# Re-ordering the first batch of a fused attention, token-mixing and gated-MLP kernel, and moving one wait and some weight splits

## The reference, cut to what matters

```
state = alpha[t] * state + k[t] v[t]^T ;  y[t] = q[t] state          # attention, per head
theta = x @ w_theta ; zr = x*cos(theta) ; zi = x*sin(theta)
u  = x + w_tok_r @ zr + w_tok_i @ zi                                 # over the 768 tokens
x2 = u + relu(u @ w_ch)
h  = relu(x2 @ w_in) ; u, v = halves of h
v_n = (v - mean(v)) / sqrt(var(v) + 1e-6)
v_s = w_spatial @ v_n + b_spatial
out = (u * v_s) @ w_out
```

## Time and profile before

| | |
|---|---|
| median of 3 runs | 617.14 us |
| the profiled execution's own time | 616.59 us |
| its span, first to last instruction | 614.9 us |
| busy: TensorE / VectorE / ScalarE / GpSimd | 586.9 / 364.6 / 223.4 / 260.4 us |
| mean granted TensorE clock | 0.994 |
| TensorE idle in all | 28.0 us |
| of that before 110 us | some 22 us, 8.9 of them the start |
| of that, waits of `angles` (395) for `xT_low`, by the view of waits | 7.6 us in 5, the longest 3.0 |

### The profile page before, as it was taken

How to read it: one execution, slowest core, us unless ns; L and a number is a source line. 1 busy time by engine, 2 the same in 40 slices (tenths; PEclk the granted TensorE clock), 3 DMA queues, 4 the chain that set the end, 5 groups by cost and what they waited for, 6 DMA issues and landing times.

```text
span 614.9 us, 11189 instructions
## 1 busy us (share of the span) xinstructions
PE 586.9 (95%) x4608; PEld 556.3 (90%) x4608; DVE 364.6 (59%) x564; ACT 223.4 (36%) x411; POOL 260.4 (42%) x208
## 2 busy tenths in 40 slices
PE   3898898999999999999999999899999999999998
PEld 3687788999999999999999989898999899989997
DVE  5799688687667876877643347537233723372132
ACT  2555454443353433433443216414131323142110
POOL 5656397554353434643513036636113611362130
PEclk9999999999999999999999999799999999999999
DMA  8652111133131311421123190200220020002002
GB/s 315 219 202 102 65 65 66 66 111 122 48 121 66 104 65 66 150 80 57 51 103 116 46 341 1 77 1 2 77 78 2 1 78 1 1 0 78 0 2 78
DMA packets 20259, 49.54 MB, mean 81 GB/s; under 512 B 1648, under 2 KB 15216, under 8 KB 19696
## 3 DMA queue, kind: packets, MB, share of 16 engines
q1 hardware_dynamic: 20208, 48.81, 22.8%
HBM read 39.37 MB, written 9.44 MB: 79 GB/s over the span
## 4 chain that ended last, share of the span: by engine, by line
PE 79%; DVE 8%; ACT 4%; POOL 3%; issue 2%; DMA 2%; SPq 0%; DVEq 0%; ACTq 0%; POOLq 0%
PE psY L413 20%; PE psY L532 6%; PE psC L445 6%; PE psC L395 5%; PE psS L532 4%; PE psF L532 4%; PE psY L506 4%; PE psS L346 3%; PE psF L374 3%; PE psC L532 2%; PE psY L516 2%; PE psS L506 2%; PE psF L496 2%; DVE akq L780 2%; DVE after L771 2%
## 5 line engine op out<-in xcount | busy, mean ns | idle before, releaser
L986 POOL TENSOR_TENSOR z_lo<-cos_sin,z_hi 128x768 fp32r<-128x768 f32 x23 | 43.0, 1869 | 107.6 <-ACT z_hi L627 107.5
L1056 POOL TENSOR_TENSOR gated_lo<-u_gated,gated_hi 128x384 fp32r<-128x384 f32 x32 | 32.4, 1012 | 126.7 <-ACT gated_hi L731 126.6
L780 DVE TENSOR_TENSOR_SCAN akq<-akq,rtotal 128x516 f32<-128x516 f32 x24 | 57.1, 2381 | 0.9
L413 PE MATMUL psY<-tok_r_hi,z_hi 128*128 128x384 f32 x141 | 51.1, 362 | 2.1 <-POOL tok_i_lo L980 1.5
L969 POOL TENSOR_TENSOR akq<-akq,after 128x512 f32<-128x512 f32 x24 | 44.4, 1848 | 9.0 <-DVE after L771 7.4
L413 PE MATMUL psY<-tok_i_lo,z_hi 128*128 128x384 f32 x141 | 47.3, 335 | 0.0
L413 PE MATMUL psY<-tok_i_hi,z_lo 128*128 128x384 f32 x141 | 47.3, 335 | 0.0
L413 PE MATMUL psY<-tok_r_hi,z_lo 128*128 128x384 f32 x141 | 47.2, 335 | 0.0
L413 PE MATMUL psY<-tok_i_hi,z_hi 128*128 128x384 f32 x141 | 47.2, 335 | 0.0
L413 PE MATMUL psY<-tok_r_lo,z_hi 128*128 128x384 f32 x141 | 47.1, 334 | 0.0
L731 ACT ACTIVATE gated_hi<-u_gated 128x384 fp32r<-128x384 f32 x32 | 16.8, 525 | 82.5 <-DVE u_gated L920 82.5
(11 more groups left out here) (222 smaller groups left out, 1753.3 us busy)
## 6 DMA issues: line engine op xcount, KB each, us to landing
akq<-akq SPq DMA_DIRECT2D x23, 770.0 KB, 4.4
v<-v_in SPq DMA_DIRECT2D x24, 192.0 KB, 4.8
x_dram<-u_f SPq DMA_DIRECT2D x8, 576.0 KB, 3.7
x_raw<-x_dram SPq DMA_DIRECT2D x4, 1152.0 KB, 5.2
out<-ot SPq DMA_DIRECT2D x24, 192.0 KB, 1.9
raw_tok_r<-w_tok_rT SPq DMA_DIRECT2D x6, 384.0 KB, 7.7
raw_tok_i<-w_tok_iT SPq DMA_DIRECT2D x6, 384.0 KB, 8.9
raw_sp<-w_spT SPq DMA_DIRECT2D x1, 2304.0 KB, 9.2
```

Of the source, the lines that this page charges most:

```text
L413: mm = pe.matmul(psY[:, j, 0:HALF], Z[s][l][:, q, tile(j)], W[m][:, s, half(h)], start=(s == 0 and q == 0 and n == 0), stop=(s == CHUNKS - ...
L780: dve.tensor_tensor_scan(ALPHA[s], ALPHA[s], rtotal[:, 1:], rtotal[:, 0:1], ALU.mult, ALU.add).then_inc(decayed, 1)
L986: pool.tensor_tensor(Z[c][1][:], trigs[g % 2][:], f(Z[c][0][:]), ALU.subtract).then_inc(z_lo, 1)
L1056: pool.tensor_tensor(GA[1][:, j, half(h)], ug[h][:, j], f(GA[0][:, j, half(h)]), ALU.subtract).then_inc(g_lo, 1)
```

## The change

- First batch, VectorE: `update_state` goes ahead of `reduce_angle`, and `xT_low` ahead of `multiply_z`.
- First batch, ScalarE: `xT_high` goes ahead of `sines`, `keep_xT` ahead of `z_high`.
- First batch from chunk 1 on, GpSimd: queries are scaled before keys, so that both scalings stand behind both scans. `scores` also waits for the keys now.
- First batch, TensorE: one third of the token unit stands ahead of `transpose_x`, two thirds behind it.
- The token weights' parts 6 to 11 are split one chunk earlier (chunks 5, 6, 7 in place of 6, 7, 8), and w_ch is split ahead of the parts of its chunk.
- First MLP batch: the wait for the bias moves from ahead of all moments to the first `gate`, the moments of tiles 0 and 1 and the first `norm` go ahead of the last three `make_x2`, and all six rows of the spatial weights get their low part on VectorE (before, the last two on GpSimd).

```diff
-SPLITS = ((0, 1), (2,), (3,), (4,), (5,), (), (6, 7), (8, 9), (10, 11)) + ((),) * (BATCH * CHUNKS)
+SPLITS = ((0, 1), (2,), (3,), (4,), (5,), (6, 7), (8, 9), (10, 11)) + ((),) * (BATCH * CHUNKS)
...
                 pe.wait_ge(q_scaled, g + 1)
+                pe.wait_ge(k_scaled, g + 1)
...
                 attend(c)
-                token_mix(FIRST_UNITS[c])
+                token_mix(FIRST_UNITS[c], (0,))
                 transpose_x(c)
+                token_mix(FIRST_UNITS[c], (1, 2))
...
                         pe.wait_ge(vn_lo, b * CHUNKS + s + 1)
-                        if s < SP_VECTOR:
-                            pe.wait_ge(sp_lo, s + 1)
-                        else:
-                            pe.wait_ge(sp_lo_end, s + 1 - SP_VECTOR)
+                        pe.wait_ge(sp_lo, s + 1)
...
                 for i in SPLITS[c]:
                     tok_high(i)
+                xT_high(c)
                 if c:
                     sines(c - 1)
-                xT_high(c)
+                keep_xT(c)
                 if c:
                     z_high(c - 1)
-                keep_xT(c)
...
-                    for i in SPLITS[g]:
-                        tok_high(i)
                     if g == CHUNKS:
                         act.wait_ge(ch_in, 16)
                         act.activation(WC[0][:], raw_ch[:], ACT.Copy).then_inc(ch_hi, 1)
+                    for i in SPLITS[g]:
+                        tok_high(i)
...
                 if c:
                     decay_keys(c + 1)
                     decay_queries(c + 1)
-                    reduce_angle(c - 1)
                 update_state(c)
                 if c:
+                    reduce_angle(c - 1)
+                xT_low(c)
+                if c:
                     multiply_z(c - 1)
-                xT_low(c)
...
                 dve.wait_ge(gi_relu, n + 1)
+                if n == 0:
+                    dve.wait_ge(bias_in, 16)
...
             make_u(HALVES * b + 1)
+            find_moments(0, 0)
+            find_moments(0, 1)
+            norm(0, 0)
             for m in range(CT):
                 make_x2((HALVES * b + 1) * CT + m, last_banks[m])
 
-            dve.wait_ge(bias_in, 16)
             for b in range(BATCH):
-                find_moments(b, 0)
-                for i in range(1, CHUNKS):
+                if b:
+                    find_moments(b, 0)
+                for i in range(1 if b else 2, CHUNKS):
                     find_moments(b, i)
                     norm(b, i - 1)
                 norm(b, 5)
                 if b == 0:
-                    for c in range(SP_VECTOR):
+                    for c in range(CHUNKS):
...
                 if c:
+                    scale_queries(c + 1)
                     scale_keys(c + 1)
-                    scale_queries(c + 1)
                 for i in SPLITS[c]:
                     tok_low(i)
...
-                    for i in SPLITS[g]:
-                        tok_low(i)
                     if g == CHUNKS:
                         pool.wait_ge(ch_hi, 1)
                         pool.tensor_tensor(WC[1][:], raw_ch[:], f(WC[0][:]), ALU.subtract).then_inc(ch_lo, 1)
+                    for i in SPLITS[g]:
+                        tok_low(i)
...
                 if b == 0:
-                    for c in range(SP_VECTOR, CHUNKS):
-                        pool.wait_ge(sp_hi, c + 1)
-                        pool.tensor_tensor(WS[1][:, c, :], raw_sp[:, c, :], f(WS[0][:, c, :]),
-                                           ALU.subtract).then_inc(sp_lo_end, 1)
```

More of the change, by code:

```diff
@@ L41 @@
 VSLOTS = 3
-SP_VECTOR = 4
 SEG = P + 1
@@ L203, in build @@
         in_in, sp_in, out_in, bias_in = sems("in_in sp_in out_in bias_in")
-        in_hi, in_lo, sp_hi, sp_lo, sp_lo_end, out_hi, out_lo = sems("in_hi in_lo sp_hi sp_lo sp_lo_end out_hi out_lo")
+        in_hi, in_lo, sp_hi, sp_lo, out_hi, out_lo = sems("in_hi in_lo sp_hi sp_lo out_hi out_lo")
         x2_in, x2_hi, x2_lo = sems("x2_in x2_hi x2_lo")
```

## The result

The changed kernel takes **620.69 us** (median of 20 runs, 617.78 to 621.99) against 616.63 (20 runs, 615.31 to 619.04): ratio 1.0058, 95% interval 1.0045 to 1.007, so slower by 0.6%. The profiled execution spans 619.6 us, 4.7 more than before. The 20 runs fall in two groups: ten have a mean granted clock of 0.992 or more and a median of 618.9 us, and ten have 0.989 or less and a median of 621.6, the profiled one (621.42, 0.986) among them. The forecast was 619.0.

The account below looks back on a forecast made before the run. VectorE was taken to bound the first batch, with TensorE busy 95% of the span. 616.59 + 8.3 (first part) - 6.4 (MLP) gave 618.5, put at 619.0 us because the profiled run lies 0.55 below the median; range 612.5 to 623.5.

Parts of the forecast that it names:

- The rule that the second comer waits for the whole instruction: VectorE and GpSimd: whichever comes second waits for the other's whole instruction, if VectorE's operands are all in SBUF.
- The cycle: First batch, chunks 2, 3 and 4: the period between masks grows from 10.33 to 12.3 us.
- Chunk 1's narrow case: First batch: chunk 1's clamp, at 25.9, comes just behind the subtraction started at 25.80; next mask 1.4 us later.
- Second scan: VectorE, first batch: with no scaling beside it, the second scan takes 1.23 us against 2.10, saving 0.87.
- Thirds cost nothing: TensorE, first batch: a third of a unit ahead of the transposes costs nothing; idle before chunk 5's angles shrinks to 1.
- Parts 6 and 7: GpSimd, chunk 5: token parts ahead of chunk 4's z subtraction make unit (0,4) start at 81.5, +7.9 us.
- Chunks 6 to 8: Some waits vanish (+7.0 us); u's late split makes the channel product wait 3.5 us; unit (1,2)'s 1.27 wait goes.
- The MLP: MLP's start: earlier copies remove the spatial-weight waits and the clock's fall, -6.4 us.
- 8.3 us at that point: Unit (1,2), after chunks 6 to 8: 7.0 + 2.9 - 1.3, rounded down, makes TensorE 8.3 us later.
- the 2.95 us ahead of 70.28 did not lower the clock: TensorE, before chunk 5's angles: an earlier 2.95 us idle gap without a clock fall, cited against the clock rival.
- The rival of the clock: First batch: clock falls at TensorE's gaps, costing 3 to 4 us each; 622 once, 625 twice; chance 0.25.
- Sign: Whole kernel: no change within 0.5% (614.1 to 620.2 us) at 0.40, slower 0.40, faster 0.20.

Follow-up runs that it names:

- e4: The changed kernel with GpSimd waiting, ahead of its token subtraction in chunks 1 to 5, until that chunk's clamp is done: 617.16 us, ratio 1.0009.
- e11: The kernel before with the change's MLP part and TensorE's units in thirds, nothing else: 612.18 us, ratio 0.9925.
- e10: The kernel before with the change's MLP part, token parts 6 to 11 a chunk earlier and w_ch ahead of them, old engine orders: 612.84 us, ratio 0.994.
- e1: The kernel before with the MLP part of the change alone: 611.10 us, ratio 0.991.
- e5: The changed kernel with 28 idle transposes on TensorE ahead of unit (0,4) and 24 ahead of the first channel product: 616.89 us, ratio 1.0008.
- e6: The kernel before with the change's MLP part and GpSimd's queries-then-keys order (with the wait for scaled keys): 610.97 us, ratio 0.9912.
- e3: The changed kernel with token parts 6 to 11 and w_ch split where they were before: 615.13 us, ratio 0.9976.
- e8: The kernel before with the change's MLP part and the new TensorE, ScalarE and VectorE orders in chunk 5 alone: 608.72 us, ratio 0.988.

## Why the prediction was right or wrong, point by point

- **The rule that the second comer waits for the whole instruction**: right. 34.04 + 1.29 is the undisturbed scan, the clamp ended 0.21 us behind the subtraction, and with the subtraction held (e4) it took 0.36.
- **The cycle**: 12.3 forecast, 12.33 measured. Chunk 1's narrow case went as forecast too (clamp at 25.64, subtraction from 25.38); chunk 5's mask came at 66.83 for 67.2.
- **Second scan**: taken as 1.23, measured 1.29. The clamps came at 1.79 for some 2.0. The Trainium skill's count (VectorE: DVE Perf Modes, on the TRN2 errata), 0.6, is not what this instruction takes, so the row rightly decided.
- **Thirds cost nothing**: right within what e11 can tell. Angles of chunk 5 at 74.34 for 74.7, idle 0.7 for 1.
- **Parts 6 and 7**: unit (0,4) forecast at 81.5, measured 81.06. That the same move costs at most 1.7 in the old order (e10) was not said.
- **Chunks 6 to 8**: the wait ahead of the channel product was forecast as 3.5 and was 2.9; the wait of unit (1,2) vanished as forecast.
- **The MLP**: -6.4 forecast, -6.41 measured between the two profiled runs.
- **The step that failed**: "8.3 us at that point". It was 11.2. The term that the sum put at nothing is the clock. Its falls added 2.7 us in unit (0,4) and 1.3 in the channel product, 4.0 in all. Against that the rest came 1.1 shorter than forecast: unit (0,4) started 0.4 earlier, the two units behind it made up 0.2 more, and the way to the channel product added 2.1 in place of 2.9, while the 0.3 that the forecast had rounded off stayed. The argument that put the clock at nothing was "the 2.95 us ahead of 70.28 did not lower the clock": one trace was read as if it were a rule, and e1 had the fall at the same place. The Trainium skill (TensorE: Matmul & The Clock Gate) says that idle time throttles the array to half rate, and the traces agree (0.50 behind 3.35 and 2.93 us of waiting); what it calls variable from run to run is the number of half-rate matmuls at a kernel's start, and these runs show the like for a later fall.
- **The rival of the clock**, at 0.25: it is what the profiled run did, and in two places. Its price was too high: 3 to 4 us for each fall, "622 once, 625 twice", where two falls cost 4.0 and the run took 621.42.
- **The time**: 619.0 forecast, 620.69 measured. That the faster half of the runs have 618.9 is in part luck and does not confirm the forecast's way to it: with the 4.0 taken off, the profiled run would be at 617.4 (an estimate), and e5, with full clock at both places, measured 616.89. The faster half lie between that and the profiled run and may still have one of the falls, which is not shown.
- **Sign**: called "no change" within 0.5%, with slower as likely (0.4 each). At +0.58% (0.45 to 0.70) the median is just on the slower side, and the bound of 0.5% lies within the interval.

## What to carry to other kernels

Where two engines shut each other out instruction by instruction, add up what each holds: here 6.0 us of GpSimd (1.84, 1.81, twice 1.18) and some 4.0 of VectorE (two scans, reciprocal, clamp, multiplication, each as long as it is undisturbed) in a cycle of 10.33. By this estimate hardly any of the cycle is left to win, so that shortening one stand only moves it to the next instruction, as e6 shows. A long independent piece of work (the state) that fills the time of another engine's reply (the sines) is not free to move: its new place left VectorE idle for 1.09 us a chunk. And split a change of many edits: one of its halves here won 5.5 us and the other lost 10, and one chunk's worth of the losing half won some 2 more.

## What the runs showed of the hardware that was not expected

- Whether TensorE's clock falls behind an idle stretch of 3 us is not settled by the length of the stretch: chunk 5's angles stood behind a gap of 2.95, 2.97 and 2.98 us in the traces of before, e1 and e10, and only e1's has the fall. It differs between runs of one program, too: e11's trace has the fall and a mean clock of 0.994, and two of its other runs have 1.000. In the change's trace the half-rate stretch at unit (0,4) was 6.8 us long and that at the channel product 3.4; matmuls of 384 columns started every 0.32 us in place of every 0.173.
- 52 idle transposes in two gaps bought 3.8 us (e5), as much as holding the subtraction (e4, 3.5) and less than moving the parts back (e3, 5.6). A wait can cost well over its length if the clock falls behind it: 3.35 us of wait and 2.7 of half rate in unit (0,4), 2.93 and 1.3 in the channel product. A fall where TensorE is not the bound (25 to 32 us in the traces of the change and of e8) showed no cost.
